# Attention stage of a fused kernel: who copies a pair's result and who copies the fourth turned tile

## What is computed

```python
q, k, v: (4, 8, 576, 64)
scores = scale * q @ k.transpose(0, 1, 3, 2)
scores = where(block_i >= block_j, scores, -1e9)        # blocks of 64
attn = exp(scores - max(scores)); attn /= attn.sum(-1) + 1e-9
x = (attn @ v) -> (2304, 512)
h = x @ w_in; x = where(h > 0, h, exp(min(h, 0)) - 1) @ w_out
out = x; for rows with x @ w_skip > 0: x + gate * relu(x @ w1[e]) @ w2[e]
```

## Time and profile before

| what | us |
|---|---|
| time, median of 3 runs | 789.53 (789.12 to 789.80) |
| profiled execution, its own time | 789.39 |
| its span (first to last instruction) | 787.6 |
| one pair in the loop | 9.09 |
| PE busy in the span | 759.1 (96%) |
| DVE busy | 522.7 (66%) |
| ACT busy | 348.1 (44%) |
| POOL busy | 244.7 (31%) |

### The profile page before, as it was taken

The page is one execution under the profiler, slowest core; times in us unless marked ns, Lnnn a source line. Parts: engine busy times, 40 slices in busy tenths (PEclk is TensorE's granted clock), DMA queues, the critical chain, the costliest instruction groups (busy, mean ns, idle before and its releaser), DMA issues.

```text
span 787.6 us, 15597 instructions
## 1 busy us (share of the span) xinstructions
PE 759.1 (96%) x5188; PEld 641.6 (81%) x5189; DVE 522.7 (66%) x1328; ACT 348.1 (44%) x830; POOL 244.7 (31%) x238
## 2 busy tenths in 40 slices
PE   5999999999999999999999999999998999999995
PEld 4777777688998888988988988998876777878884
DVE  4888888854337974985797598436755997367342
ACT  4888888644322223223222322224452784446231
POOL 4888887944501200210121021000112231222211
PEclk9999999999999999999999999999999999999998
DMA  9556667561323122101210200502334898164000
GB/s 164 134 143 160 162 162 188 150 199 58 143 79 109 45 60 91 50 21 50 72 41 0 91 22 28 214 1 81 116 115 126 273 344 298 47 232 150 34 15 10
DMA packets 101062, 88.17 MB, mean 112 GB/s; under 512 B 63812, under 2 KB 78532, under 8 KB 100880
## 3 DMA queue, kind: packets, MB, share of 16 engines
q1 hardware_dynamic: 95584, 81.89, 34.8%
q0 software_dynamic: 3056, 5.00, 1.9%
q10 hardware_dynamic: 2368, 0.59, 0.4%
HBM read 72.26 MB, written 18.34 MB: 115 GB/s over the span
## 4 chain that ended last, share of the span: by engine, by line
PE 86%; ACT 5%; DVE 3%; issue 2%; DMA 1%; SPq 1%; DVEq 1%; POOL 0%; ACTq 0%; POOLq 0%
PE out_ps L1755 12%; PE h_ps L1755 12%; PE out_ps L1757 12%; PE out_ps L1756 12%; PE h_ps L1756 12%; PE h_ps L1757 12%; PE o_ps L684 5%; ACT prob L541 3%; PE s_ps L668 3%; PE t_ps L593 2%; PE out_ps L1891 1%; PE s_ps L663 1%; ACT pt L525 1%; DMA w_raw<-in_moe_w_out_dram 1%; PE tr_ps L1856 1%
## 5 line engine op out<-in xcount | busy, mean ns | idle before, releaser
L1580 ACT ACTIVATE ex<-h_ps 128x384 f32<-128x384 f32 x96 | 47.3, 493 | 273.0 <-PE h_ps L1757 273.0
L1755 PE MATMUL h_ps<-xt_hi,wi_hi 128*128 128x384 f32 x384 | 131.8, 343 | 0.6 <-DVE ex L1413 0.6
L1756 PE MATMUL h_ps<-xt_lo,wi_hi 128*128 128x384 f32 x384 | 129.7, 338 | 0.0
L1757 PE MATMUL h_ps<-xt_hi,wi_lo 128*128 128x384 f32 x384 | 129.7, 338 | 0.0
L1410 DVE TENSOR_SCALAR ex<-ex 128x384 f32<-128x384 f32 x96 | 37.6, 392 | 132.2 <-ACT ex L1580 130.8
L1755 PE MATMUL out_ps<-wo_hi,gt 128*128 128x512 f32 x288 | 114.6, 398 | 0.1
L1757 PE MATMUL out_ps<-wo_hi,gt 128*128 128x512 f32 x288 | 113.9, 396 | 0.0
L1756 PE MATMUL out_ps<-wo_lo,gt 128*128 128x512 f32 x288 | 113.3, 393 | 0.0
L541 ACT ACTIVATE prob<-s_ps,negmax 128x128 f32<-128x128 f32 (+2 forms) x144 | 77.8, 554 | 12.5 <-DVE negmax L399 11.6
L1288 DVE CUSTOM_DVE_ANT_0 x2t<-x,w_raw 128x512 bf16<-128x512 f32 x108 | 82.7, 805 | 0.4
L1178 POOL TENSOR_TENSOR xt_lo<-x_raw,xt_hi 128x384 fp32r<-128x384 f32 x20 | 28.3, 1413 | 158.3 <-ACT xt_hi L1597 158.0
(11 more groups left out here) (185 smaller groups left out, 1624.5 us busy)
## 6 DMA issues: line engine op xcount, KB each, us to landing
w_raw<-in_moe_w_dram SPq DMA_DIRECT2D x56, 512.0 KB, 5.4
raw_qk<-in_q_dram SPq DMA_DIRECT2D x32, 144.0 KB, 3.3
attn_t<-attn_sb SPq DMA_DIRECT2D x16, 288.0 KB, 2.2
x_raw<-attn_t SPq DMA_DIRECT2D x24, 192.0 KB, 2.5
w_raw<-recip_rows SPq DMA_DIRECT2D x48, 96.0 KB, 2.9
out_dram<-x SPq DMA_DIRECT2D x18, 256.0 KB, 2.6
x_rows<-x SPq DMA_DIRECT2D x18, 256.0 KB, 2.8
v<-in_v_dram SPq DMA_DIRECT2D x32, 128.0 KB, 2.8
```

The costliest lines, as they stand in the source:

```text
L1580: act.activation(ex[:, f % 2], h_ps[:, f % 2, 0:NB], ACT.Exp).then_inc(ex_done, 1)
L1755: pe.matmul(dst, stat[0], mov[0], start=start, stop=False, skip_group_check=True)
L1756: pe.matmul(dst, stat[0], mov[1], start=False, stop=False, skip_group_check=True)
L1757: return pe.matmul(dst, stat[1], mov[0], start=False, stop=stop, skip_group_check=True)
```

## The change

`final` moves from VectorE to ScalarE for all pairs but the last two, whose `final` stays on VectorE. On ScalarE it stands behind `exp(now, 2)` and ahead of the copy of tile 3. ScalarE's `turned_third` copies only the first of the two banks (halves=(0,)) while there is a pair now; the second bank is copied by VectorE in a new `turned_third`, behind `row_max(now, 3)` and ahead of the copy of tile 1. It has a semaphore of its own, t3b_out, and the turn of tile 2 on PE, which writes the same two banks, waits for both.

```diff
@@ vector
+        def turned_third(n, i):
+            wait(dve, t3_done, n + 1)
+            dve.tensor_copy(pt[i][:, :, 0:FULL, 3 * P + D:4 * P],
+                            t_ps[:, 1, :].rearrange("p (h j w) -> p h j w", h=2, w=D)).then_inc(t3b_out, 1)
@@ vector, step
-            if older and now:
-                final(*older)
             if now:
                 row_max(now[0], 3)
+                if past:
+                    turned_third(*past)
                 turned_halves(*now, 1, o_turns, t1_done, t1_out)
@@ scalar
+        def final(n, i):
+            wait(act, pv_done, n + 1)
+            wait(act, stored[1 - i], 16 * ((n + i) // 2))
+            act.activation(attn_sb[:, :], o_ps[:, O0:O0 + S], ACT.Copy).then_inc(out_done, 1)
-        def turned_third(n, i):
+        def turned_third(n, i, halves=(0, 1)):
             wait(act, t3_done, n + 1)
-            for s in range(2):
+            for s in halves:
@@ scalar, step
-            if past:
-                turned_third(*past)
+            if older and now:
+                final(*older)
+            if past and now:
+                turned_third(*past, halves=(0,))
             if now:
                 exp(*now, 3)
@@ tensor, step
-            copied = [(t3_out, now[0])] if past else [(prep_out, 6), (tail_q_out, 2)]
+            copied = [(t3_out, now[0]), (t3b_out, now[0])] if past else [(prep_out, 6), (tail_q_out, 2)]
```

More of the change, by code:

```diff
@@ L192, in attention_engines @@
     out_done = sem("out_done")
+    t3b_out = sem("t3b_out")
     wi_in = sem("wi_in")
@@ L553, in step @@
         def step(kk, i):
-            now, past, after = pair(kk, i), pair(kk, i, -1), pair(kk, i, 1)
+            now, past, older, after = pair(kk, i), pair(kk, i, -1), pair(kk, i, -2), pair(kk, i, 1)
             if after:
```

## The result

| | before | after |
|---|---|---|
| time, median (lowest to highest), us | 789.58 (788.61 to 790.34) | 792.72 (792.20 to 794.52) |
| profiled execution, its own time; span | 789.39; 787.6 | 792.69; 791.0 |
| PE, DVE, ACT busy | 759.1, 522.7, 348.1 | 760.3, 524.8, 349.4 |
| one pair in the loop (mean of nine, pair 4 to 13) | 9.09 | 9.40 |

What follows compares the result with a forecast made beforehand. The prediction took PE's chain of short links as the bound, with PE newly waiting for VectorE's copies. Loop and pair 13 gave 2.8 us, pair 14 0.65: some 3.5 over 789.39, so 792.9 us, range 791.0 to 794.7.

Steps and rivals of the forecast that it cites:

- the maximum's gain of 0.17: VectorE, loop: without the result's copy ahead of it, the maximum of tile 3 starts 0.17 us earlier (69.48, not 69.65).
- ScalarE's unused 0.24: ScalarE, loop: the exponentials of tile 3 start 0.24 us earlier, but PE's waits for VectorE leave that gain unused.
- nothing from the result's copy in the loop: ScalarE, loop: the result's copy hides in 0.97 us of idleness ahead of tile 3's copy and costs nothing.
- The first rival: Loop: new copy hidden, ScalarE's shorter path decides, if it takes under 0.39 us of VectorE; faster, 786.9 us; chance 0.05.
- the pair, 0.21 forecast: Loop: PE's mixed turn starts 0.21 us later a pair (73.60, not 73.39); pairs 2 to 12 sum to 2.4 us.
- the release of PE by VectorE: PE's waits for VectorE's copies: a matmul starts some 0.06 us behind the instruction that releases it.
- the two rooms: Slack before PE waits for VectorE's copies: 0.09 us at the turn of q and k, 0.22 at the mixed turn.
- the prediction's own upper case: Upper end of the slower forecast: 0.30 us a pair in the loop, 4.6 us in all, 794.0 us.
- pairs 0 to 1 at nothing: First two pairs: no result to copy yet and no near wait for VectorE, so no cost counted.
- pair 13 at 0.43: VectorE's row in pair 13: its whole delay of 0.43 us counts, as VectorE reaches pair 14's maxima late.
- pair 14 at 0.65: Pair 14: ScalarE has no idleness, so PE's turn of tile 1 waits 0.95 us and the mixed turn comes 0.65 later.
- this goes to the end: Behind pair 15: loads and feed-forward matmuls shift with its mixed turn, so the whole 3.5 us reaches the end.

Runs made afterwards that it cites:

- putting the copy back: Changed kernel with the result's copy of steps 14 and 15 back on VectorE, the loop as changed: 792.85 us, ratio 1.0053.
- the result's copy alone: Kernel before with the result's copy moved to ScalarE, which keeps both copies of tile 3; VectorE has no new copy: 790.08 us, ratio 1.0002.
- the better share: Changed kernel, but VectorE copies only 128 columns of tile 3's second bank, ScalarE the rest; result of steps 14 and 15 on VectorE: 789.11 us, ratio 0.9999.
- the same with the multiplications cut: The better share with VectorE's multiplications ahead of pairs 14 and 15 cut to one column: 787.29 us, ratio 0.9984; whole time not comparable with uncut kernels.

## Why the prediction was right, and where its terms were off

**Right: what bounds the pair.** The new copy of 0.60 against the maximum's gain of 0.17 (0.14 by the runs), ScalarE's unused 0.24, and nothing from the result's copy in the loop are as forecast. In the trace the wait of scores 0 for the exponentials is gone and ScalarE waits at the last tile's maximum. Thinned and doubled, the copy moves the period by just the time that it takes on VectorE. The first rival, that the copy is hidden, held for a copy under 0.39 us; the measured limit is 0.29, and the copy takes 0.60.

The Trainium skill's rule that was weighed (page "VectorE: DVE Perf Modes", section "The TRN2 errata") gave 0.66 for this copy; the row says 0.60 from start to start (72.38 to 72.98), and 0.68 long. For the step of a running row the start-to-start distance of the trace was the right price; what a copy releases starts behind its recorded end.

**Mis-sized: the pair, 0.21 forecast, 0.32 measured.** The step that failed is the release of PE by VectorE, taken as 0.06 us from an end of matmuls to a VectorE start. The other direction is slower: VectorE's copy of tile 2 ends at 75.32 and the mixed turn starts at 75.42 (0.10). In the other of the loop's two pairs it is 0.18:

```profile
64.86 1.01 DVE L444 COPY pt<-t_ps 128x384 f32<-128x384 f32 x2
```
```profile
66.05 0.65 PE L608 MATMUL t_ps<-ident,prob 64*128 64x64 f32 x14
```

The copy ends at 65.87 (VectorE's timeline), and the turn starts at 66.05 (PE's). These are the two lengths of the period, 9.37 and 9.45 by turns. The mean of 0.14 is 0.08 over the 0.06. The same term had made the two rooms too wide: with 0.14 for the crossing the second is 73.39 - 73.11 - 0.14 = 0.14 and not 0.22, which with the 0.14 of the earlier maximum is the measured break-even. Of the first (0.15 from the copy's end at 71.51 to the turn at 71.66) next to nothing is left. Two small pieces make up the rest: the maximum's start to the copy's end is 4.08 and not 4.06, and the way from the mixed turn to the end of the next scores 3 is 5.14 or 5.15, for 5.13 before. Together 0.11 or so, by 11 pairs 1.1 us more than the 2.4 forecast: 3.50. That is a little over the prediction's own upper case (0.30 a pair), and not for its reason: it had put the extra 0.09 down to VectorE's copy costing its full length, and it doesn't.

**Wrong: pairs 0 to 1 at nothing.** 0.42 us stand there already at pair 2. 0.18 of them come before the first pair's fourth maximum (15.57 before, 15.75 after), where the change has no instruction; the rest is within what the first steps scatter by from kernel to kernel (below). I count it as no effect of the change; one trace of each kernel can't show more.

**Wrong: pair 13 at 0.43.** It gave -0.08 (142.51 to 146.34 is 3.83, after 3.91). The prediction read the kernel before there as it stood, with its multiplications of 2.11 us, and did not ask why two like instructions of 0.55 took that long. They took 1.02 in the changed kernel, since the shift had brought them to a place where GpSimd stood idle, and a microsecond of lateness was gone.

**Wrong in its mechanism: pair 14 at 0.65.** It gave 0.34. PE's turn of tile 1 was to wait 0.95 us for the result's copy; it stood still 0.21, since that lateness of VectorE was gone. Then VectorE's row was the longer way, and putting the copy back changed nothing (9.66 against 9.70). In the kernel with the result's copy alone, where the multiplications are stretched, the forecast mechanism is there: the turn stood still 0.78 us, and the step is 1.31 us longer (10.48 against 9.17), twice the forecast 0.65.

**Wrong: "this goes to the end".** Of the 4.17 us at the mixed turn of pair 15 0.5 came back up to 192 us and 0.3 more in the part with the experts. The first part has a trace behind it. In the kernel before the chain ran through the load of w_out, for which ScalarE waited:

```profile
163.61 1.28 ACT L1645 ACTIVATE wo_hi<-w_raw 128x512 fp32r<-128x512 f32 x2 [1.99 <-DMA w_raw<-in_moe_w_out_dram]
```

In the changed kernel ScalarE makes these copies without a wait for the load, and the chain stays on PE from 155 us through the hand-over (ScalarE's timeline):

```profile
165.51 1.66 ACT L1660 ACTIVATE wo_hi<-w_raw 128x512 fp32r<-128x512 f32 x3
```

So the load no longer ends the chain there; SP issued it 3.5 us later (157.45 and 160.96), where the mixed turn came 4.2 later. The prediction had allowed some 0.6 us either way for its landing. No run varies it, so its part in the 0.5 is read and not shown, and what gives back the last 0.3 wasn't tried.

So the sum: start 0.4 more than forecast, the loop 1.1 more, pairs 13 and 14 0.5 and 0.3 less, the rest of the program 0.8 less. The forecast of the total, 3.5 us against 3.4, owes much to these cancelling. The sign and the range don't: each of the kernels that have the new copy at full width is slower, with an interval wholly over 1.

## What to carry to other kernels

A copy that leaves a waiting engine is worth its wait, and one that joins an engine that others wait for costs its start-to-start time in full: measure the room from both releases in the timeline, and price the crossing from engine to engine in the direction in which it is used. Before a copy is divided between two engines by halves, work out the share at which the second one breaks even (here 0.29 us of VectorE, 128 of 512 columns and not 512). And when an instruction takes three times its usual length in the trace of before, find what it collides with first; any shift, for better or worse, may undo or bring that.

## What the runs showed of the hardware that was not expected

**A two-input VectorE instruction beside a two-input one of GpSimd** took 1.64 instead of 0.55 us, and ended 0.4 us behind GpSimd's. The better share gained 0.9 us in the loop and lost 1.06 at one such place.

**The crossing from VectorE to a waiting matmul** took 0.10 to 0.18 us at the mixed turn; from matmuls to VectorE 0.05. The turn of tile 2 with three waits started 0.26 behind the last, with two 0.11.

**TensorE's granted clock at the start.** In some traces the clock falls for about 2 us around 24 to 28, in others not, though the kernels hardly differ up to there. The better share and the same with the multiplications cut are the same program up to pair 14. The windows view of the better share (start and end, length, then busy time of PE, PEld, DVE, ACT, POOL with their instructions, granted clock, DMA share, GB/s):

```profile
18.00:22.00 4.00, 2.50 (x50) 2.07 (x46) 3.63 (x11) 4.00 (x16) 3.74 (x4) 1.00 0.14 39
...
24.00:26.00 2.00, 2.00 (x14) 1.60 (x12) 1.47 (x4) 2.00 (x6) 2.00 (x2) 0.50 0.65 118
```

The same with the multiplications cut:

```profile
18.00:22.00 4.00, 2.50 (x50) 2.07 (x46) 3.63 (x11) 4.00 (x16) 3.74 (x4) 1.00 0.17 46
...
24.00:26.00 2.00, 1.98 (x36) 1.73 (x33) 2.00 (x5) 2.00 (x6) 2.00 (x2) 1.00 0.56 107
```

0.50 is 1.2 of 2.4 GHz, and 14 matmuls stand where the other has 36. Ahead of it PE had been busy 2.50 us of 4 in both, so what decides it stays open. The step from the fourth maximum of pair 1 to that of pair 2 takes 9.9 to 10.0 us with the dip and 9.0 to 9.4 without (the kernel with the copy made twice, whose pair is 10.0 anyway, aside), and the changed kernel's profile has the dip as the one before does. It is about as large as the whole gain of the better share, which is why the verdicts here rest on the period of the loop and on the intervals, not on single times.
